# An attention and two MLPs on one core: the second head pair's loads of batch 0 are issued ahead of the first two pieces of MLP weights

## The chip, the cores and the metric

The kernel runs on one core of a Trainium2 chip. The metric is the device time of the whole program in microseconds (us); the kernel before takes 1157.22 us as the median of three runs (1156.96 to 1162.31).

## The reference

The inputs are q, k and v of shape (4 batches, 8 heads, 576 tokens, 64), all fp32.

```
out_up    = repeat(attention(mean-pooled q, k, v over 4 tokens), 4)   # 144 tokens
out_local = attention(q, k, v) with |row - col| < 4
x   = (out_up + out_local) as 2304 tokens x 512
h   = relu(x @ w_in)                 # w_in 512 x 2048
x   = (s * h * h + b) @ w_out        # first MLP, w_out 2048 x 512
out = ((x @ w_a) * (x @ w_b)) @ w2   # second MLP, d_ff 1536
```

Both attentions scale by 1/8 and use a softmax with its row maximum taken off and 1e-9 added to the sum.

## The kernel before

**Stages.** Heads are taken in pairs, so a batch has four pairs. The kernel first computes the attention of batch 0 alone (four pairs, overlapped with one another), and beside it brings in the weights of the first MLP and splits them. Then it runs the first MLP of batch m beside the attention of batch m+1, for all four batches, and last the second MLP. Each matrix product of the MLPs is three fp32r matmuls of high and low parts (hi·hi, hi·lo, lo·hi), and this is why weights have to be split: `hi` is the weight rounded to fp32r, `lo` the remainder.

**The first stage as steps.** The attention of one pair is laid out over steps `at` = 0 to 16, and pair p starts at step 11·p. At steps 0 to 3 TensorE turns q and k of the pair (L383, four transposes a step, read from `nat`), and ScalarE copies the result to `qT` and `kT` (L586). VectorE sums groups of four tokens (`pooledT`, L743). There are six score blocks j = 0 to 5 (two pooled, L407, and four local, L415), starting at steps 4, 6, 8, 9, 10 and 11. For block j, VectorE adds the mask (L755, local blocks), takes the maximum (L757) and the shift (L759); a step later ScalarE takes the exponentials (L598); another step later VectorE inverts the sums (L768, L770); GpSimd multiplies by them (L923); TensorE turns the result (L432, L436), ScalarE copies it (L607), TensorE multiplies with v (L446, L454), and VectorE takes the output (L777, L788). GpSimd also sums v over groups (L914, L917) at step 1 of a pair. Every engine runs its list of steps strictly in the written order.

**The weight pieces.** The first MLP's weights come in 16 pieces of 128 x 1024 fp32 (512 KB), through two buffers in `scratch` that alternate. A piece c is taken in two moves. At step 3(c+1), ScalarE (L622) and GpSimd (L928) each copy half of it to `hi`, after what they have to do for the attention in that step; both first wait for the piece's DMA. At step 3(c+1)+1 VectorE writes `lo` (L807), also at the end of its step, after waiting for both halves of `hi`. So piece 0 is wanted at step 3 by ScalarE and GpSimd and at step 4 by VectorE, pieces 1 and 2 at steps 6 and 9, and piece 3 at step 12.

**SP's queue.** All DMAs are issued by SP, in one written order. `load_pair(i, p)` issues 12 DMAs: four for q and k (L256), after waiting until the previous pair's four turns are done, two for v in groups (L259), and six for v in windows (L269). `load_piece(c)` issues one DMA (L279 for w_in, L284 for w_out); from c = 2 on it first waits until piece c-2 is wholly split (L273 to L275), because both share a buffer. The order of batch 0 before is: identity, pair 0, mask and two scalars (L294 to L296), pieces 0 and 1, pair 1, pieces 2 to 5, pair 2, pieces 6 to 9, pair 3, pieces 10 to 13, pieces 14 and 15, then pair 0 of batch 1. VectorE waits for the mask and both scalars before its first step. The first MLP begins on TensorE only when all 16 pieces are split and batch 0's attention is done.

The lines that hold the casts in place are, on ScalarE:

```
                if at % 3 == 0 and 0 < at // 3 <= NPIECE:
                    split_w_hi(at // 3 - 1)
```

on GpSimd the same, and on VectorE:

```
                if at % 3 == 1 and 0 < at // 3 <= NPIECE:
                    split_w_lo(at // 3 - 1)
```

Of the kernel before, what the change touches and what calls it, by code (L numbers as in the profile page):

```python
# [62 lines left out]
def build(nc, q, k, v, w_in, w_out, s, b, w_a, w_b, w2, mask_in, identity, out, o_dram):  # L63
# [6 lines left out]
    with stack:  # L70
# [177 lines left out]
        def _(sp):  # L248
            def load_pair(i, p):
                n = PAIRS * i + p  # L250
                past(sp, turn_ready, TURNS * n)
                for t, a in enumerate((q, k)):
                    for half in range(2):
                        dst = nat[:, t, half].rearrange("g r (h d) -> g r h d", h=2)
                        src = a.rearrange("b h (f g r) d -> b f g r h d", f=2, r=POOL)
                        sp.dma_start(dst, src[i, half, :, :, 2 * p:2 * p + 2, :]).then_inc(nat_in, 16)  # L256
                past(sp, vd_ready, n)
                for half in range(2):
                    sp.dma_start(vnat[:, half], groups_src(v, i, half, p)).then_inc(vnat_in, 16)  # L259
                if alone(i) and p == 0:  # L260
                    sp.wait_ge(vwin_clear, 1)
                past(sp, o_ready, NG * (n - 1))
                for w in range(NW):
                    lo_row = HALO if w == 0 else 0
                    hi_row = WK - HALO if w == NW - 1 else WK
                    t0 = WQ * w - HALO
                    src = v[i, 2 * p:2 * p + 2, t0 + lo_row:t0 + hi_row, :].rearrange("h t d -> t h d")
                    dst = vwin[lo_row:hi_row, p % 2, w, :].rearrange("t (h d) -> t h d", h=2)
                    sp.dma_start(dst, src).then_inc(vwin_in[p % 2], 16)  # L269

            def load_piece(c):
                if c >= 2:
                    sp.wait_ge(w_hi, c - 1)  # L273
                    sp.wait_ge(w_hi_pool, c - 1)
                    sp.wait_ge(w_lo, c - 1)  # L275
                if c < W1F // PIECE:
                    kd, part = divmod(c, FF1 // PIECE)
                    src = w_in[kd * P:(kd + 1) * P, part * PIECE:(part + 1) * PIECE]
                    sp.dma_start(piece_sb[:, c % 2, :], src).then_inc(piece_in[c % 2], 16)  # L279
                else:  # L280
                    f = (c - W1F // PIECE) * (PIECE // DM)
                    src = w_out[f * P:(f + PIECE // DM) * P, :].rearrange("(f p) m -> p f m", p=P)
                    dst = piece_sb[:, c % 2, :].rearrange("p (f m) -> p f m", m=DM)
                    sp.dma_start(dst, src).then_inc(piece_in[c % 2], 16)  # L284
# [9 lines left out]
            sp.dma_start(mask[:], mask_in).then_inc(consts_in, 16)  # L294
            sp.dma_start(s_col[:], s.partition_broadcast(P)).then_inc(consts_in, 16)
            sp.dma_start(b_col[:], b.partition_broadcast(P)).then_inc(consts_in, 16)  # L296
            load_piece(0)
            load_piece(1)
            for p in range(1, PAIRS):
                load_pair(0, p)  # L300
                for c in range(4 * p - 2, 4 * p + 2):
                    load_piece(c)
            load_piece(NPIECE - 2)
            load_piece(NPIECE - 1)
# [677 lines left out]
```

## Time and profile before

| | |
|---|---|
| median of three runs | 1157.22 us (1156.96 to 1162.31) |
| span of the profiled execution | 1150.5 us |
| own time of the profiled execution | not listed beside its span; the median of the runs is 6.7 us above the span |
| mean granted TensorE clock | 0.998 |
| TensorE matmuls busy | 1094.9 us (95%) |
| VectorE, ScalarE, GpSimd busy | 461.8, 422.7, 113.8 us |
| DMA | 52.43 MB, 91086 packets |
| the batch-0 stage | from 0 to about 111 us of the span |

All times of rows are microseconds from the start of the span. A line of the timeline gives start, duration, engine, source line, operation, and the output and input tensors, with the idle time of the engine just before it and what ended that idle time. SPq is SP's issuing of DMAs, so its duration is the issue and not the transfer. In the chain of waits each piece is the work, or the transfer in flight, that released the next one.

### The profile page before, as it was taken

Reading aid. Unit: us, or ns where it says so; the run is one execution under the profiler, and the core shown is the slowest. Engines: PE = TensorE matmul, PEld = TensorE weight load, DVE = VectorE, ACT = ScalarE, POOL = GpSimd, SP = SyncE. Lnnn points to the kernel's source line nnn. Section 1 sums busy time; section 2 is a strip of 40 time slices with the busy share of each in tenths; the row PEclk is TensorE's granted clock in tenths of the full one; section 3 lists DMA queues with packets and bytes.
Section 4 is the critical chain, followed back from the end, with each engine's and each line's share of the span. In section 5 each row is a group of like instructions: output and inputs, shape, how many; then the busy total and the mean of one; then the engine's idle time right before and its main releaser. Section 6 shows DMA issues by size and latency. Waiting matters only on the chain.

```text
span 1150.5 us, 19365 instructions
## 1 busy us (share of the span) xinstructions
PE 1094.9 (95%) x7048; PEld 1003.4 (87%) x7048; DVE 461.8 (40%) x1078; ACT 422.7 (37%) x1191; POOL 113.8 (10%) x149
## 2 busy tenths in 40 slices
PE   3887999999999999999999999999999999999998
PEld 3676899998989988999899998999989899999997
DVE  3766644455555455545533344421121211211211
ACT  3654544454445445445433343321121221211211
POOL 2433111210121112011100000000000000000000
PEclk9999999999999999999999999999999999999999
DMA  6443110112012101110040016201010010010000
GB/s 167 119 130 98 43 43 20 45 44 63 8 36 64 43 24 42 44 47 18 2 131 1 22 30 184 83 19 38 1 55 0 0 55 0 22 33 0 27 0 27
DMA packets 91086, 52.43 MB, mean 46 GB/s; under 512 B 59808, under 2 KB 84000, under 8 KB 91008
## 3 DMA queue, kind: packets, MB, share of 16 engines
q1 hardware_dynamic: 91008, 51.42, 16.1%
q8 instruction: 46, 0.75, 0.3%
q14 instruction: 32, 0.26, 0.1%
HBM read 41.97 MB, written 9.44 MB: 45 GB/s over the span
## 4 chain that ended last, share of the span: by engine, by line
PE 89%; SPq 3%; ACT 3%; DVE 3%; issue 1%; DMA 1%; DVEq 0%; ACTq 0%
PE bank L543 25%; PE bank L480 19%; PE bank L492 18%; PE bank L553 12%; PE bank L454 4%; PE bank L415 3%; PE bank L436 2%; PE bank L446 2%; PE bank L407 2%; PE bank L383 2%; SPq L256 1%; SPq L269 1%; PE bank L432 1%; ACT sm L598 1%; DVE lo L807 1%
## 5 line engine op out<-in xcount | busy, mean ns | idle before, releaser
L543 PE MATMUL bank<-x_hi,hi 128*128 128x384 f32 x576 | 193.9, 337 | 8.1 <-DVE prod L894 4.1
L543 PE MATMUL bank<-x_hi,lo 128*128 128x384 f32 x576 | 193.7, 336 | 0.0
L543 PE MATMUL bank<-x_lo,hi 128*128 128x384 f32 x576 | 193.4, 336 | 0.0
L480 PE MATMUL bank<-hi 128*128 128x288 f32 x512 | 160.7, 314 | 1.0 <-ACT scratch L649 1.0
L894 DVE TENSOR_TENSOR prod<-bank,a_sb 128x384 f32<-128x384 f32 x72 | 40.2, 558 | 293.4 <-ACT a_sb L711 293.4
L492 PE MATMUL bank<-g_hi,hi 128*128 128x288 f32 x512 | 157.8, 308 | 0.0
L480 PE MATMUL bank<-lo,hi 128*128 128x288 f32 x512 | 152.1, 297 | 0.0
L492 PE MATMUL bank<-g_lo,hi 128*128 128x288 f32 x512 | 151.8, 296 | 0.0
L480 PE MATMUL bank<-hi,lo 128*128 128x288 f32 x512 | 151.8, 296 | 0.0
L492 PE MATMUL bank<-g_hi,lo 128*128 128x288 f32 x512 | 150.9, 295 | 0.0
L830 DVE SCALAR_TENSOR_TENSOR scratch<-scratch,s_col 128x288 f32<-128x288 f32 x128 | 66.4, 519 | 189.4 <-ACT scratch L649 189.4
L711 ACT ACTIVATE a_sb<-bank 128x384 f32<-128x384 f32 x72 | 35.4, 492 | 290.8 <-PE bank L543 290.8
L649 ACT ACTIVATE scratch<-bank 128x288 f32<-128x288 f32 x128 | 52.7, 411 | 184.1 <-PE bank L480 184.0
L543 PEld LDWEIGHTS bank<-x_hi,hi 128*128 128x128 f32 x576 | 108.2, 188 | 13.7 <-ACT x_hi L644 6.0
L543 PEld LDWEIGHTS bank<-x_lo,hi 128*128 128x128 f32 x576 | 108.2, 188 | 3.1
L543 PEld LDWEIGHTS bank<-x_hi,lo 128*128 128x128 f32 x576 | 108.2, 188 | 0.0
L923 POOL TENSOR_TENSOR sm<-sm,den 96x306 f32<-96x306 f32 (+1 forms) x96 | 65.6, 684 | 423.7 <-DVE den L770 423.7
L480 PEld LDWEIGHTS bank<-hi 128*128 128x128 f32 x512 | 97.3, 190 | 6.1 <-issue 4.6
L492 PEld LDWEIGHTS bank<-g_hi,hi 128*128 128x128 f32 x512 | 96.6, 189 | 5.3 <-issue 4.8
L480 PEld LDWEIGHTS bank<-lo,hi 128*128 128x128 f32 x512 | 97.5, 190 | 0.0
L480 PEld LDWEIGHTS bank<-hi,lo 128*128 128x128 f32 x512 | 97.1, 190 | 0.0
L492 PEld LDWEIGHTS bank<-g_lo,hi 128*128 128x128 f32 x512 | 96.7, 189 | 0.0
(64 smaller groups left out, 1719.2 us busy)
## 6 DMA issues: line engine op xcount, KB each, us to landing
nat<-in_q SPq DMA_DIRECT2D x32, 144.0 KB
nat<-in_k SPq DMA_DIRECT2D x32, 144.0 KB
vnat<-in_v SPq DMA_DIRECT2D x32, 144.0 KB
o_transposed<-scratch SPq DMA_DIRECT2D x8, 576.0 KB, 3.5
o_raw<-o_transposed SPq DMA_DIRECT2D x6, 768.0 KB, 4.7
out<-y SPq DMA_DIRECT2D x18, 256.0 KB, 2.0
scratch<-in_moe_w_in SPq DMA_DIRECT2D x8, 512.0 KB, 4.4
scratch<-in_moe_w_out SPq DMA_DIRECT2D x8, 512.0 KB, 3.5
```

The lines of the kernel that those rows point to most:

```text
L383: mm = nc.tensor.transpose(turn_bank(i, t)[:, r * GH:(r + 1) * GH], nat[:, t // 2, t % 2, r, :], ident[0:GH, 0:GH])
L415: mm = nc.tensor.matmul(s_bank(i, j)[0:WQ, u * WK:(u + 1) * WK], qT[rows, w * WQ:(w + 1) * WQ], kT[rows, w * WQ:w * WQ + WK], start=True, ...
L454: mm = nc.tensor.matmul(o_bank(i, j)[e * D:(e + 1) * D, u * WQ:(u + 1) * WQ], vwin[:, p % 2, GW * half + u, e * D:(e + 1) * D], pts[:, j % ...
L480: mm = nc.tensor.matmul(HB[:, 0:HALF], wi(w, kd, f % F1), xs(x, h)[:, kd], start=(kd == 0 and n == 0), stop=(kd == KD - 1 and n == 2))
L492: mm = nc.tensor.matmul(ACC[o][:, 0:HALF], wo(w, f % F1, o), g[:, f % GB, :], start=(f % F1 == 0 and n == 0), stop=(f % F1 == F1 - 1 and n ...
L543: mm = nc.tensor.matmul(dst[:, 0:CH2], block2(w, f, j * KD + kd), x[:, kd, :], start=(kd == 0 and n == 0), stop=(kd == KD - 1 and n == 2))
L553: mm = nc.tensor.matmul(ACC[tt], x[:, f % GB, tt * P:(tt + 1) * P], rows2(w, f), start=(f == 0 and n == 0), stop=(f == F2 - 1 and n == 2))
L649: nc.scalar.activation(relu[:, f % 2, :], HB[:, 0:HALF], ACT.Relu).then_inc(r_ready, 1)
L711: nc.scalar.activation(a_sb[:, f % 2, :], HB[:, 0:CH2], ACT.Copy).then_inc(a_ready, 1)
L830: nc.vector.scalar_tensor_tensor(sq[:, f % 2, :], relu[:, f % 2, :], s_col[:, 0:1], relu[:, f % 2, :], ALU.mult, ALU.mult).then_inc(q_read ...
L894: nc.vector.tensor_tensor(prod[:, f % 2, :], SB[:, 0:CH2], a_sb[:, f % 2, :], ALU.mult)\
L923: nc.gpsimd.tensor_tensor(sm_view(j), sm_view(j), spread(den, j), ALU.mult).then_inc(p_ready, 1)
```

## The change

SP issues the twelve DMAs of batch 0's pair 1 before those of pieces 0 and 1. Nothing else moves: pieces 2 to 5 still follow, then pair 2, and no other engine's list changes.

```diff
             sp.dma_start(b_col[:], b.partition_broadcast(P)).then_inc(consts_in, 16)
-            load_piece(0)
-            load_piece(1)
             for p in range(1, PAIRS):
                 load_pair(0, p)
-                for c in range(4 * p - 2, 4 * p + 2):
+                for c in range(4 * p - 2 if p > 1 else 0, 4 * p + 2):
                     load_piece(c)
             load_piece(NPIECE - 2)
             load_piece(NPIECE - 1)
```

## Rows read from the trace of the kernel before

**Rows 1.** The page: busy time, share and instructions of each engine.
```profile
PE 1094.9 (95%) x7048; PEld 1003.4 (87%) x7048; DVE 461.8 (40%) x1078; ACT 422.7 (37%) x1191; POOL 113.8 (10%) x149
```

**Rows 2.** Chain of waits, 0 to 45 us: start, duration, what.
```profile
11.10 0.43 SPq L279
...
14.82 3.12 SPq L256
...
23.24 4.11 DMA scratch<-in_moe_w_in
27.34 0.02 issue
27.37 0.63 ACT hi L622
28.00 1.09 ACT sm L598 x6
...
30.66 0.69 PE bank L383 x4
...
32.37 0.91 ACT sm L598 x5
```

**Rows 3.** Timeline of SP's issues, from 0 to 50 us.
```profile
1.18 1.84 SPq L256 DMA_DIRECT2D nat<-in_q  x2
...
9.74 0.38 SPq L294 DMA_DIRECT2D mask<-band_mask  x1
...
38.39 1.68 SPq L256 DMA_DIRECT2D nat<-in_q  x2
...
47.09 2.26 SPq L279 DMA_DIRECT2D scratch<-in_moe_w_in  x2
```

**Rows 4.** Timeline of TensorE, the last turns of pair 0 and first pooled scores.
```profile
9.66 1.26 PE L383 MATMUL bank<-ident,nat 72*128 72x72 f32 x8 [0.29 <-ACT qT L586]
16.84 1.25 PE L407 MATMUL bank<-pooledT 64*72 64x144 f32 x8 [5.92 <-DVE pooledT L743]
```

**Rows 5.** The loads of w_in pieces (L279), issue to landing.
```profile
DMA to landing us min/median/max: 3.6/4.4/6.7
```

**Rows 6.** Timeline of ScalarE, 16 to 33 us.
```profile
16.64 0.63 ACT L622 ACTIVATE hi<-scratch 128x512 fp32r<-128x512 f32 x1 [4.99 <-DMA scratch<-in_moe_w_in]
18.97 0.38 ACT L598 ACTIVATE sm<-bank,shift 72x144 f32<-72x144 f32 x1 [1.71 <-DVE shift L759]
...
27.37 0.63 ACT L622 ACTIVATE hi<-scratch 128x512 fp32r<-128x512 f32 x1 [2.56 <-DMA scratch<-in_moe_w_in]
```

**Rows 7.** Timeline of VectorE, 18 to 32 us.
```profile
18.60 0.34 DVE L759 TENSOR_SCALAR shift<-mx 72x2 f32<-72x2 f32 x1
18.85 1.21 DVE L807 TENSOR_TENSOR lo<-scratch,hi 128x1024 fp32r<-128x1024 f32 x1
...
26.81 0.17 DVE L759 TENSOR_SCALAR shift<-mx 96x3 f32<-96x3 f32 x1
28.12 1.63 DVE L807 TENSOR_TENSOR lo<-scratch,hi 128x1024 fp32r<-128x1024 f32 x1 [1.14 <-POOL hi L928]
29.67 0.15 DVE L768 TENSOR_SCALAR den<-den 96x3 f32<-96x3 f32 x1
...
30.95 1.11 DVE L759 TENSOR_SCALAR shift<-mx 96x3 f32<-96x3 f32 x1
```

**Rows 8.** Timeline of GpSimd, 27 to 31 us.
```profile
27.97 0.69 POOL L923 TENSOR_TENSOR sm<-sm,den 96x306 f32<-96x306 f32 x1
...
30.76 1.27 POOL L914 TENSOR_TENSOR vnat<-vnat 72x512 f32<-72x512 f32 x1
```

**Rows 9.** Chain of waits, 97 to 119 us: the end of the stage.
```profile
109.26 1.24 DVE lo L807
110.50 0.50 issue
110.99 0.71 PE bank L383 x4
```

## The prediction

> **What bounds the kernel now.** I read the page first: TensorE's matmuls are busy for 95% of the span [rows 1], so a saving or a loss must reach TensorE's own order of work. The part that the diff touches lies in the first 111 us, where it does: TensorE's first MLP cannot start before the last piece of weights is split, and the chain ends this stage on VectorE's last `lo`, at 109.26, which releases TensorE at 110.99 [rows 9]. Whatever delays that point delays the end by as much, because behind it TensorE is nearly always busy and nothing there waits on a clock of its own.
>
> Then I read the chain of waits of the stage from its start. Up to 23.24 it runs through SP's issues one behind the other; then it is the flight of piece 2, 4.11 us; then ScalarE's cast of it at 27.37, exponentials, pair 1's turns at 30.66, exponentials at 32.37 [rows 2]. After that it is compute, with one more walk through SP. So at first sight SP's order matters and the nearest wait is for piece 2, not for pair 1.
>
> The engines' timelines give the slack. ScalarE waits 4.99 us for piece 0, casts it at 16.64, and waits 2.56 us for piece 2 [rows 6]. VectorE is not late for piece 0: it starts the first `lo` at 18.85, right behind its own shift, 1.58 us after the cast ended (16.64 + 0.63 = 17.27). For piece 2 it waits 1.14 us [rows 7].
>
> **The change part by part.** *Nothing is removed or added*: the same DMAs, casts and waits. Pair 1's twelve issues move 0.96 us earlier and two piece loads move later, past twelve issues.
>
> *Pair 1's loads earlier* buys nothing. They are first used at pair 1's turns at 30.66, and those follow ScalarE and TensorE work in the chain, not a DMA [rows 2]; I count 0, and since no row shows a wait for pair 1's data a gain is excluded. Their own first wait, the turns of pair 0, is over at 9.66 + 1.26 = 10.92, before the 11.10 at which SP gets there [rows 2, 4], so it costs 0 too.
>
> *When piece 0 is issued.* SP is free at 11.10. A pair's load took 9.74 - 1.18 = 8.56 us for pair 0 and 47.09 - 38.39 = 8.70 for pair 2 [rows 3], but from 12.05 (two piece issues behind 11.10) to 23.24, 11.19 us, for pair 1, with a single issue of 3.12 us in it, where its neighbours take about 0.9 [rows 2, 3]. That issue stood behind the 1 MB of two pieces just asked for; afterwards these are not ahead of it. I take the mean of pairs 0 and 2, 8.65 us: piece 0 is issued at 19.75 instead of 11.10. Bounds: 8.56 and 11.19, so 19.66 to 22.29.
>
> *When it lands.* Piece 2 is the same case, a piece straight behind a pair's twelve loads: 4.11 us [rows 2]. Piece 0 today takes 16.64 - 11.10 = 5.54 us, and the piece loads lie between 3.6 and 6.7 [rows 2, 5, 6]. I take 4.11, since the queue ahead of it will be that of piece 2: landing at 23.86. Bounds 3.6 and 5.54.
>
> The DMA page of the Trainium skill (DMA: Bandwidth & Descriptors, section "Anatomy of one DMA") fits a transfer as 2.0 us plus bytes over 436 GB/s, which for 512 KB is an estimate of 3.2 us. By it piece 0 would land 0.9 us sooner, and the sum below would be 0.9 us less. The row is above it, and no w_in piece of this trace was below 3.6; the sum goes by the row.
>
> *Who is held by it.* ScalarE runs in its written order, so at step 3 it stands in the cast of piece 0 until 23.86, and the exponentials of block 0 (18.97 today) are queued behind it. GpSimd stands in its own half. VectorE has its shift ready at 18.94 but stands in `lo` of piece 0, behind which are queued the sums of block 0 and the maxima of block 1. TensorE waits for block 0's exponentials. The cast takes 0.63, so it ends at 24.49, and VectorE follows 0.11 later, as it follows today's cast of piece 2 (28.00 to 28.12): 24.60 against 18.85. That is a delay of **5.75 us** at VectorE's first `lo` [rows 6, 7]. ScalarE's is 24.49 against 18.97, 5.5 us, so VectorE leads.
>
> *What absorbs part of it.* From 18.85 to the shift that starts at 26.81, VectorE is occupied nearly throughout and feeds ScalarE and TensorE, so all of it moves by 5.75. Next stands `lo` of piece 2. Today VectorE waits 1.14 us for that piece. Afterwards piece 2 can be issued once piece 0 is split: 24.60 + 1.21 = 25.81, about 25.9, landing at 30.0 by 4.11. ScalarE gets to it at 27.37 - 2.56 + 5.75 = 30.56, so the cast doesn't wait, and ends at 31.2. VectorE comes at 26.81 + 0.17 - 0.09 + 5.75 = 32.64 (its instructions start about 0.09 before the listed end of the one ahead [rows 7]), so its wait of 1.14 us is gone. It starts `lo` of piece 2 at 32.64 against 28.12: 4.52 us late.
>
> *A small gain.* That `lo` takes 1.63 us today and lies on GpSimd's multiplication at 27.97 to 28.66; the first one took 1.21 [rows 7, 8]. Afterwards the multiplication depends on sums that are ready at about 30.9 and is over by 31.6, so I take 1.21 - 1.63 = -0.42 (bounds -0.42 and 0). Delay behind it: 4.52 - 0.42 = **4.1 us**.
>
> Here a rule bears: SBUF — State Buffer of the Trainium skill, section "Who interferes with whom", says that a VectorE instruction with two SBUF inputs and a GpSimd one that reads SBUF exclude each other for the whole instruction. The 1.63 against 1.21 agrees. Without the rule, taking the 1.63 as it is, the sum would be 4.5 us.
>
> *Who carries the 4.1 on.* The chain before went through ScalarE's cast (which moves by only 31.2 - 28.0 = 3.2 us) to pair 1's first turn. The exponentials of block 5 at about 32.1 come behind both ScalarE's own order and the shift of 30.95 + 1.11 = 32.06 [rows 2, 7]. That shift moves by 4.1, so VectorE's path is the one that is last and the end moves by 4.1. Its 1.11 us, overlapped by GpSimd's sum at 30.76 [rows 8], stays as it is: both follow the same sums. Everything later (pairs 2 and 3, their waits on turns, the pieces' waits on splits) hangs on this point, and no later event in the stage has an origin outside it. I count 0 for later slack; bounds: 0, and 1.5 us given back.
>
> **Sum**: 8.65 (later issue) - 1.43 (landing 4.11 for 5.54) - 1.58 (slack of VectorE at piece 0) + 0.11 (following the cast) - 1.14 (wait for piece 2 gone) - 0.08 (start before listed end: 28.12 - 26.98 is 1.14, 28.12 - 26.89 is 1.23) - 0.42 = 4.1 us. Against the profiled span: 1150.5 + 4.1 = 1154.6. The runs' median is 6.7 us above that span, and nothing of it lies in the changed stage, so 1157.22 + 4.1 = **1161.3 us**, 0.35% slower. I treat 0.5% (5.8 us) as about what a measurement can tell from no change; so this is likely a real loss, but inside that bound.
>
> **Rivals.**
>
> *A. The long issue stays.* If the 3.12 us is not owed to the two pieces but to what else is in the queue (the mask and scalars are just ahead in both orders), pair 1 still takes 11.19 us, 2.5 more than in the sum: 4.1 + 2.5 = 6.6, 1163.8. With a landing of 5.54 it is 8.1, 1165.3. For it: that issue is in this very pair. Against: pair 0 and pair 2 have twelve issues without it.
>
> *B. The wait is hidden.* If pair 0's work could run on around piece 0, or later slack took it all, 1157.2. For it: the stage has idle time on every engine. Against: the cast is ahead of the exponentials in ScalarE's order, and each engine's order is fixed. Partial absorption, down to +2, belongs here. That the order of transfers doesn't change in effect (both sets are in flight together) would also end here, but 8.65 us of issue lie between.
>
> *C. Faster: SP's own stream is what counts.* The chain to 23.24 is SP's, and its 3.12 us issue is in it. If this shrinks to 0.9, SP arrives at piece 2 some 2.5 us sooner, the waits of 2.56 and 1.14 us for it vanish, and VectorE gains 1.14 + 0.42 = 1.6 us: 1155.6. It decides if piece 0 can land by 18.1, where VectorE's slack ends, and it is even at a landing of 19.8. The issue itself is not before 19.66, so only a transfer overtaking SP's issues, or ScalarE not standing in the cast, would bring it.
>
> **How the numbers follow.** Forecast (2.5 to 5.8 us later) 0.68; A (above 5.8) 0.20; B (from +2.5 down to 0) 0.10; C 0.02. The range: the lower end is issue and landing at their lower bounds (-0.1 - 0.5) with 1.5 us given back, 4.1 - 2.1 = +2.0, or 1159.2, widened to 1158.7 for the scatter of 0.3 and more between the runs; the upper end is A with a part of the longer landing, +7.6, or 1164.8. Chances: faster by over 0.5% 0.01 (C's 1.6 us would not reach it), within 0.5% 0.78 (forecast, B, most of C), slower by over 0.5% 0.21 (A and a little of the forecast's tail).
>
> **What would show it.** After: pair 1's issues from 11.10 in about 8.7 us without an issue of 3 us; piece 0 issued near 19.8; ScalarE's first cast near 23.9 with about 12 us idle ahead of it, ended by the DMA; VectorE's first `lo` near 24.6; no wait for piece 2 on ScalarE or VectorE; that `lo` near 32.6 and 1.2 us long; TensorE's first MLP matmuls about 4 us later than 111; the rest unchanged. A first cast before 20 would prove me wrong, and so would one past 26 or a start of the MLP moved by under 2 us.

## The result and the profile after

The changed kernel takes 1160.65 us (median of 20 runs, 1155.99 to 1165.59) against 1156.33 us of the kernel before (20 runs). The ratio is 1.0038 with a 95% interval of 1.0021 to 1.0054: 4.3 us slower, clear of noise, and less than 0.5%. Forecast were 4.1 us. The interval reaches from 2.4 to 6.2 us, so the run times confirm the sign and the rough size; the terms of the sum are checked in the profiles.

The numbers of the pages hardly differ from [rows 1]; line numbers behind the changed lines are two lower after. The page of the kernel after, busy time by engine:

```profile
PE 1096.5 (95%) x7048; PEld 1005.0 (87%) x7048; DVE 463.5 (40%) x1078; ACT 422.5 (37%) x1191; POOL 114.6 (10%) x149
```

The chain of waits of the kernel after, 0 to 45 us, answers to [rows 2]:

```profile
11.11 0.84 SPq L256
...
13.67 0.80 SPq L256
...
17.33 1.19 SPq L269
...
19.01 4.10 DMA scratch<-in_moe_w_in
23.11 0.05 issue
23.16 0.62 POOL hi L926
...
23.88 1.23 DVE lo L805
25.10 0.51 DVE den L766
```

The reader should see that the flight on the chain is now that of piece 0, at 19.01, where before it was that of piece 2, at 23.24, and that pair 1's fourth q/k issue takes 0.80 us where it took 3.12. Behind the flight come GpSimd's cast and VectorE's `lo` on the chain.

ScalarE's and VectorE's timelines of the kernel after, answering to [rows 6, 7]:

```profile
23.13 0.63 ACT L620 ACTIVATE hi<-scratch 128x512 fp32r<-128x512 f32 x1 [11.34 <-DMA scratch<-in_moe_w_in]
23.67 0.36 ACT L596 ACTIVATE sm<-bank,shift 72x144 f32<-72x144 f32 x1
...
30.17 0.61 ACT L620 ACTIVATE hi<-scratch 128x512 fp32r<-128x512 f32 x1
```
```profile
16.90 0.17 DVE L757 TENSOR_SCALAR shift<-mx 72x2 f32<-72x2 f32 x1
23.88 1.23 DVE L805 TENSOR_TENSOR lo<-scratch,hi 128x1024 fp32r<-128x1024 f32 x1 [6.81 <-POOL hi L926]
25.02 0.58 DVE L766 TENSOR_SCALAR den<-den 72x2 f32<-72x2 f32 x1
...
32.34 1.22 DVE L805 TENSOR_TENSOR lo<-scratch,hi 128x1024 fp32r<-128x1024 f32 x1
...
34.77 1.11 DVE L757 TENSOR_SCALAR shift<-mx 96x3 f32<-96x3 f32 x1
```

ScalarE idles 11.34 us for piece 0, and VectorE has its shift ready at 17.07 and stands for 6.81 us. ScalarE and VectorE don't wait for piece 2 any more: neither the cast at 30.17 nor the third `lo` at 32.34 has idle time ahead of it. (GpSimd idles 0.33 us for it, and its cast is over by 29.65, well ahead of that `lo`.) The end of the stage, from the chain of the kernel after, answering to [rows 9]:

```profile
112.51 1.24 DVE lo L805
113.75 0.45 issue
114.20 0.71 PE bank L381 x4
```

TensorE starts 3.2 us later than in the profile of before. The spans differ by more, 1156.1 against 1150.5. Most of the rest is the clock: over 60-us stretches the granted TensorE clock reads 1.00 except for single stretches at 0.97, of which the kernel before has one and this one has two. A stretch of 0.97 holds a short dip to the lower of the clock's two levels, 1.2 GHz instead of 2.4: in the kernel before the 4 us from 276 to 280 alone read 0.57. Of the kernel before, one such stretch and its neighbour (columns: the stretch and its length, busy time and instructions of each engine, granted clock, DMA share, GB/s):

```profile
240.00:300.00 60.00, 57.57 (x431) 52.38 (x430) 33.88 (x95) 30.89 (x108) 9.55 (x14) 0.97 0.15 38
300.00:360.00 60.00, 60.00 (x464) 54.91 (x463) 29.24 (x76) 27.18 (x83) 9.56 (x12) 1.00 0.15 37
```

and of the kernel after:

```profile
120.00:180.00 60.00, 58.01 (x433) 52.83 (x432) 31.18 (x87) 28.40 (x95) 8.38 (x11) 0.97 0.17 41
...
660.00:720.00 60.00, 55.44 (x350) 53.71 (x349) 25.53 (x33) 22.48 (x34) 0.00 (x0) 0.97 0.31 91
```

A stretch at 0.97 is 3% of 60 us, so one more of them costs an estimated 1.8 us of the 2.4 us that are left. Comparing runs of one mean clock takes this away. At 0.998 the five runs of the kernel after have a mean of 1157.4 us, and the kernel before, in 17 runs timed later with the experiments, 1153.2: a difference of 4.2 us, though not between runs timed together.

### The profile page after: what moved, and what is told of

It reads as the page before. It is cut to its first block, busy times and chain, and to the rows that moved or that the text cites. A ratio compares the mean times of both kernels' runs of the same rounds, so it can differ in the third digit from the quotient of the medians.

```text
span 1156.1 us, 19365 instructions
## 1 busy us (share of the span) xinstructions
PE 1096.5 (95%) x7048; PEld 1005.0 (87%) x7048; DVE 463.5 (40%) x1078; ACT 422.5 (37%) x1191; POOL 114.6 (10%) x149
## 4 chain that ended last, share of the span: by engine, by line
PE 89%; DVE 3%; ACT 3%; SPq 2%; DMA 2%; issue 1%; DVEq 0%; ACTq 0%; POOL 0%
PE bank L541 25%; PE bank L478 18%; PE bank L490 18%; PE bank L551 12%; PE bank L452 4%; PE bank L413 4%; PE bank L434 2%; PE bank L444 2%; PE bank L381 2%; PE bank L405 2%; SPq L256 1%; PE bank L430 1%; DVE lo L805 1%; SPq L269 1%; ACT sm L596 1%
```

## The experiments

All numbers of this table are starts on the timeline: of VectorE's `lo` of pieces 0, 3, 9 and 10, and of TensorE's first work behind the last split.

| kernel | piece 0 | piece 3 | piece 9 | piece 10 | TensorE | ratio (95%) |
|---|---|---|---|---|---|---|
| before | 18.85 | 35.93 | 70.82 | 77.53 | 110.99 | 1 |
| after | 23.88 | 39.75 | 74.65 | 80.79 | 114.20 | 1.0038 (1.0021 to 1.0054) |
| after, again | 24.23 | 40.10 | 75.01 | 82.94 | 116.36 | 1.0047 (1.0029 to 1.0064) |
| after, mask wait moved | 23.94 | 39.82 | 74.29 | 81.09 | 114.51 | 1.0040 (1.0024 to 1.0055) |
| one piece behind | 17.87 | 41.38 | 76.29 | 82.17 | 115.63 | 1.0048 (1.0028 to 1.0068) |
| casts later | 23.55 | 38.43 | 73.32 | 80.38 | 113.80 | 1.0032 (1.0012 to 1.0051) |
| only q, k ahead | 20.20 | 36.08 | 70.98 | 77.57 | 110.99 | 1.0008 (0.9985 to 1.0031) |
| before, mask wait moved | 16.92 | 34.77 | 69.75 | 77.38 | 110.80 | 0.9998 (0.9976 to 1.0020) |
| piece 2 early | 18.18 | 33.63 | 68.53 | 75.89 | 109.30 | 0.9944 (0.9924 to 0.9965) |
| both | 17.11 | 32.99 | 67.89 | 75.06 | 108.47 | 0.9960 (0.9943 to 0.9977) |
| both, and piece 10 | 16.64 | 33.31 | 68.22 | 74.41 | 107.28 | 0.9973 (0.9954 to 0.9993) |

From piece 3 to piece 9 all kernels take 34.9 to 35.0 us, but for the fourth row (34.5); from piece 10 to TensorE's start, 33.4 us, but for the last (32.9). So a kernel's loss or gain is fixed at piece 3, and the only place where it changes by much is between pieces 9 and 10 (5.9 to 7.9 us). Two of the kernels ("after, mask wait moved" and "both, and piece 10") were timed on another chip than the other experiments. Each ratio is to runs of the kernel before that were timed together with the kernel.

**The changed kernel again.**

> The changed kernel itself once more, to see how far its stages repeat. Theory: piece 0 lands at 23.1 to 23.9, TensorE's start behind the last split at 114.2 within 0.5 us, and the ratio to the kernel before 1.003 to 1.005. Rival (the 3.2 us at the end of the stage is chance of one profile): a start anywhere from 111 to 115.

It landed piece 0 at 23.48 and was 4.17 us behind at piece 3, against 3.82: that repeats. The start of TensorE doesn't: 116.36, not 114.20, outside the theory's half microsecond and above the rival's range too. Its chain shows why, 66 to 83 us:

```profile
76.89 5.28 DMA scratch<-in_moe_w_out
```

and the same flight, of piece 10 behind pair 3's loads, in the first profile of the kernel after:

```profile
76.40 3.61 DMA scratch<-in_moe_w_out
```

The end of the stage carries a scatter of some 2 us from this one flight. The reading to trust is that of piece 3.

**One piece behind.** Half of the change, as a diff against the kernel before.

```diff
             load_piece(0)
-            load_piece(1)
             for p in range(1, PAIRS):
                 load_pair(0, p)
-                for c in range(4 * p - 2, 4 * p + 2):
+                for c in range(4 * p - 2 if p > 1 else 1, 4 * p + 2):
```

> Piece 0 stays ahead of pair 1's loads, only piece 1 goes behind them. The number to look at is the start of TensorE's first work behind the last split (110.99 us before, 114.20 after). Theory (ScalarE, GpSimd and VectorE stand in their written order before a late piece): piece 0 lands near 16.6 as before, piece 1 is issued near 20.2 and lands near 24.3, VectorE's second lo starts near 25.0 instead of 21.0, and after the 1.1 us of wait for piece 2 and 0.4 us of overlap are given back, the start is 2.4 us later than before, near 113.4. Rival (only the first piece's lateness counts, later ones find slack): 111.0.

The mechanism holds and the size doesn't: the start is 4.6 us later, not 2.4, and at piece 3 the loss is 5.45 us, more than that of the whole change. SP's and ScalarE's timelines of this kernel:

```profile
13.15 3.54 SPq L256 DMA_DIRECT2D nat<-in_k  x2
...
21.76 21.24 SPq L279 DMA_DIRECT2D scratch<-in_moe_w_in  x5
```
```profile
17.12 0.63 ACT L621 ACTIVATE hi<-scratch 128x512 fp32r<-128x512 f32 x1 [5.41 <-DMA scratch<-in_moe_w_in]
27.14 0.63 ACT L621 ACTIVATE hi<-scratch 128x512 fp32r<-128x512 f32 x1 [8.44 <-DMA scratch<-in_moe_w_in]
```

With one piece ahead, three quarters of the long issue are back (the two k issues take 3.54 us, against 4.17 with two pieces ahead and 1.63 with none), so piece 1 is issued at 21.76 and not at 20.2, and its flight is 5.4 us and not 4.1. Both were mis-sized in the expectation. The 8.44 us of idle time stand at the second cast, so a late second piece is paid for as well, and the rival (only the first piece's lateness counts) falls.

**Only q and k ahead.** `load_pair` is cut in two functions, `load_qk` and `load_v`. The order, against the kernel before:

```diff
+            load_qk(0, 1)
             load_piece(0)
             load_piece(1)
-            for p in range(1, PAIRS):
+            load_v(0, 1)
+            for c in range(2, 6):
+                load_piece(c)
+            for p in range(2, PAIRS):
```

> Only the four q and k loads of pair 1 go ahead of pieces 0 and 1; its eight v loads stay behind them. Theory (VectorE has 1.6 us of slack at piece 0, and SP is then free for piece 2 some 2.5 us sooner because no 3 us issue comes up): piece 0 is issued near 14.5 and lands near 18.6, the first lo starts near 19.35, 0.5 us late, the wait of 1.14 us for piece 2 goes, and TensorE's start moves to 109.9, 1.1 us sooner than before. Rival (any lateness of piece 0 is paid in full): 0.5 to 2 us later, 111.5 to 113.

Neither: 0.15 us late at piece 3, and 110.99 at the end, as before. Piece 0 was issued at 14.26 as expected, but flew 5.2 us and landed at 19.45, so the first `lo` was 1.35 us late. The second was 1.78 late, the third 0.55 and the fourth 0.15, so the wait for piece 2 took it up. Slack of this size is there, and the rival, that any lateness is paid in full, falls. The theory's gain of 1.1 us failed because SP did not come to piece 2 sooner (22.85, against 23.24 in the kernel before): the k issues were short, but the six issues of v windows behind the two pieces took 6.44 us where they took 3.86. The hold-up had moved to them:

```profile
16.27 6.44 SPq L271 DMA_DIRECT2D vwin<-in_v  x6
```

**Casts later.** The order of loads of the changed kernel, with the casts elsewhere in the lists; the diff is against that kernel.

```diff
+                if at in (6, 8):
+                    split_w_hi((at - 6) // 2)
-                if at % 3 == 0 and 0 < at // 3 <= NPIECE:
+                if at % 3 == 0 and 2 < at // 3 <= NPIECE:
                     split_w_hi(at // 3 - 1)
```

(on ScalarE and GpSimd; VectorE's `lo` at 7 and 9 in the same way)

> The order of loads of the changed kernel; but the casts of pieces 0 and 1 stand at steps 6 and 8 and their lo at 7 and 9 of every engine's list, instead of 3, 6 and 4, 7. Theory (the cost is the place of the cast in a fixed order, in front of block 0): exponentials of block 0 run near 17.2 instead of 23.7, piece 0 still lands near 23.1, VectorE has block 1's maxima done before it, and TensorE's start is 1.5 us sooner than in the changed kernel, near 112.7. Rival (transfers of pair 1 and the pieces get in each other's way, whatever the casts' place): 114.2.

Piece 0 arrived about as late as in the changed kernel, and ScalarE had block 0's exponentials done before it, at 16.95:

```profile
22.80 0.63 ACT L620 ACTIVATE hi<-scratch 128x512 fp32r<-128x512 f32 x1 [5.03 <-DMA scratch<-in_moe_w_in]
```

The loss at piece 3 shrank from 3.82 to 2.50 us. The cast was 0.33 us earlier than in the changed kernel, so 1.0 to 1.3 us of the loss was the place of the cast in a fixed order, with the same DMAs in the same order. The other 2.5 us remain because the piece is still late at its new place: ScalarE idles 5.03 us and VectorE 4.82 us for it, and ScalarE another 0.82 us for piece 2. No run moved the casts further back. The start at 113.80 is only 0.4 us sooner than the 114.20, since the interval from piece 9 to 10 was 7.06 us here and 6.14 there.

**Mask wait moved**, in the kernel before and in the changed one.

```diff
                 if j >= POOLED:
+                    if alone(i) and p == 0 and j == POOLED:
+                        dve.wait_ge(consts_in, 48)
...
-            dve.wait_ge(consts_in, 48)
```

> The kernel before, but VectorE waits for the mask and the two scalars at its first masked block instead of at its start. Theory (SP's walk to piece 2 sets the time of the kernel before, not VectorE): the first pooled sums start near 11.7 instead of 15.4, the first lo near 17.4 instead of 18.85, and ScalarE just waits longer for piece 2, so that TensorE's start behind the last split stays at 111.0 within 0.3 us. Rival (VectorE's own chain sets it): 1.5 us sooner, 109.5.

> The changed kernel, with VectorE waiting for the mask and scalars only at its first masked block. Theory (in the changed kernel VectorE stands at its first lo for the cast of piece 0, with 6.8 us idle): the pooled sums start near 11.8 instead of 13.7, the idle time grows by as much, and the first lo (23.9) and the fourth (39.8) stay within 0.4 us. Rival (VectorE's early start counts there too): up to 1.9 us sooner at both.

In the changed kernel the first `lo` stood 9.66 us for the cast and stayed at 23.94, the fourth at 39.82: VectorE's early start buys nothing there. In the kernel before, the first `lo` came 1.9 us sooner and the third 1.2, with ScalarE still waiting 2.87 us for piece 2. These 1.2 us are not the edit's, as far as the profile shows: SP's issues ahead went quicker in this profile and reached piece 2 at 22.30 and not 23.24. The start moved by only 0.2 us, since the interval from piece 9 to 10 was 7.63 us here and 6.71 in the kernel before, and the ratio is 1.

**Piece 2 early.** If SP's walk to piece 2 bounds the kernel before, then the right thing to move is piece 2.

```diff
             load_piece(0)
             load_piece(1)
-            for p in range(1, PAIRS):
+            load_qk(0, 1)
+            load_piece(2)
+            load_v(0, 1)
+            for c in range(3, 6):
+                load_piece(c)
+            for p in range(2, PAIRS):
```

> The kernel before, but piece 2 is issued between the q,k loads and the v loads of pair 1. Theory: SP waits for the first lo until 20.1, piece 2 lands near 24.4 at the latest instead of 27.4, the waits of 2.6 and 1.1 us for it go, and TensorE's start moves from 111.0 to 109.5 (1.14 us of wait and 0.42 us of overlap). Rival (piece 2 is hidden anyway, or the later v loads are missed): 111.0 or later.

> The two edits together: VectorE's wait for the mask moved back, and piece 2 issued ahead of pair 1's v loads. Theory (each hides the other's gain): first lo near 17.4, piece 2 issued near 18.7 and landed near 22.9, TensorE's start near 108.0, 3.0 us sooner than before, and the whole 0.25% faster. Rival (no more than the second edit alone): 109.5.

Piece 2 was issued at 19.50; ScalarE's third cast and the third `lo` have no idle time ahead, and piece 3 is 2.30 us sooner, the start 1.7. Of the 2.30, 0.67 were there at the first `lo` already, from quicker issues, which leaves 1.6 for the edit. VectorE's timeline of this kernel, with the wait of [rows 7] gone:

```profile
26.22 1.23 DVE L818 TENSOR_TENSOR lo<-scratch,hi 128x1024 fp32r<-128x1024 f32 x1
```

With both edits it is 2.94 us at piece 3 and 2.5 at the start. The intervals of the two ratios overlap, and their middles stand the other way round, so that "both" beats the one edit rests on one profile of each. The times gained more than the starts did: 0.56% is 6.5 us (interval 4.0 to 8.8, six runs) beside 1.7 us at the start, and 0.40% is 4.6 us (2.7 to 6.6) beside 2.5. A part may be that the one profile of the kernel before caught a short flight of piece 10 (3.5 us, against up to 5.4 in others) and so an early start; the rest is not explained.

**And piece 10.** The same order in pairs 2 and 3, as a diff against the kernel with both edits.

```diff
             for p in range(2, PAIRS):
-                load_pair(0, p)
-                for c in range(4 * p - 2, 4 * p + 2):
+                load_qk(0, p)
+                load_piece(4 * p - 2)
+                load_v(0, p)
+                for c in range(4 * p - 1, 4 * p + 2):
```

> The two edits of the sixth kernel, and in pairs 2 and 3 too the next piece (6 and 10) is issued between the q,k loads and the v loads. Theory (the stage has one more place where SP's walk through a pair's loads is last: piece 10 behind pair 3, flights of 3.5, 3.6 and 5.3 us in three profiles, and an interval of 6.1 to 7.9 us between the tenth and eleventh lo): the tenth lo stays near 67.9, the interval shrinks to 5.9 as behind pair 2, TensorE's start is near 107.2 instead of 108.5, and it no longer scatters. Rival (ScalarE and TensorE are last there as well): 108.5.

The start came at 107.28, 3.7 us before that of the kernel before, as expected. At the mean clock of 0.998, four runs average 1149.5 us and four of the kernel before, timed together with them, 1152.5. It is faster than the kernel before and than the changed one; against "both" the ratios (0.9973 and 0.9960) don't tell the two apart. Its piece 9 to 10 took 6.19 us, and no engine waited for piece 10, whose `lo` took 1.21 us and not 1.63; one profile can't say that the scatter is gone. At piece 2 the order did not do what it does in the two kernels ahead: that load, asked for at 17.98, was in flight for 6.76 us, and ScalarE idled 1.70 us for it, so that piece 3 came 0.3 us later than in "both". Its chain of waits:

```profile
17.98 6.76 DMA scratch<-in_moe_w_in
```

So asking for a piece ahead of the v loads takes the wait away in two profiles of three.

## Why the prediction was right, step by step

- *Pair 1's loads earlier, 0*: right. No profile puts an engine's wait down to them.
- *Later issue, +8.65*: measured 19.01 - 11.10 = 7.91, which is 0.74 less and below the lower bound of 8.56. The long q/k issue is gone, as forecast, but the term was read from pairs 0 and 2, whose six v-window issues took 3.87 and 4.00 us; here they took 3.38. (Their mean is also 8.63, not 8.65.) Over all profiles pair 1's two k issues took 3.5 to 4.7 us where one or two pieces stood just ahead of its q and k (six profiles), and 1.63 where none did (five). Rival A, as a long issue without the pieces ahead, fell. Its thought that something else in the queue plays a part stays open: at pairs 2 and 3 a piece stands just ahead as well, and there the two k issues took 1.6 to 2.4 us, and once 3.2.
- *Flight, 4.11*: measured 4.12 here and 4.6 in the second profile. That it can be 5.4 with one piece ahead, or 5.2 behind q and k alone, was within the bounds (3.6 to 5.54) but not foreseen, and the 6.76 us of piece 2 in the last kernel lie beyond them. The fit that the prediction quotes from the Trainium skill (DMA: Bandwidth & Descriptors, section "Anatomy of one DMA") is given there for DMAs issued by GpSimd, and these are SP's. The estimate of 3.2 us from it is below the flight of every piece straight behind a pair's loads that ScalarE waited for (3.5 to 5.4 us in ten profiles), so going by the row was right.
- *VectorE's slack and the following of the cast, -1.58 + 0.11*: the landing moved by 6.49 us and the first `lo` by 5.03, so -1.46: right.
- *Not in the sum*: the pieces now land close together, and GpSimd's cast of piece 1 lies on VectorE's sum (0.58 us for 0.15 before, the row at 25.02). That is +0.43 at the second `lo`, which the prediction put at nothing.
- *Wait for piece 2 gone, -1.14 and -0.08*: the delay fell from 5.46 to 4.22, so -1.24. Right.
- *The shorter third `lo`, -0.42*: 1.22 for 1.63, and the delay fell to 3.82 at piece 3. The trace agrees with the rule of the Trainium skill (SBUF — State Buffer, section "Who interferes with whom"): GpSimd's multiplication (30.75 to 31.44) was over before this `lo`.
- *The sum*: 7.91 - 1.42 - 1.46 + 0.43 - 1.24 - 0.40 = 3.82, against 4.1. That it comes so near is in part luck: the issue term was 0.74 us too large and the 0.43 us left out offset more than half of it.
- *Nothing later*: right from piece 3 to 9 (34.90 us against 34.89). Between pieces 9 and 10, 0.6 us were given back in the first profile and 1.2 us lost in the second, by chance of a flight. The prediction saw one more walk through SP behind 45 us, but counted nothing for it, on the ground that no later event has an origin outside this point; the flight of piece 10 is such an event. Its sum fits the point that repeats, and the end only within that scatter.
- *Rival B* (hidden) is excluded by the 3.8 us at piece 3 and by the interval. *Rival C* pointed at the right resource and the wrong move: SP's walk did bound the kernel before, and taking piece 2 through it sooner gained 1.6 us at piece 3 (the changed kernel lost 3.8 there).
- *What lies around the span, 6.7 us*: that was a profiled run at a high mean clock beside a median at a lower one. The profiled run of the kernel after took 1157.86 for a span of 1156.1, so 1.8 us lie around it, and the rest of the 6.7 is between runs. The forecast of 1161.3 stands on the 1157.22 of three runs; over 20 runs the kernel before has 1156.33.

## What to carry to other kernels

A load that no one is waiting for is not improved by being asked for sooner, and it is paid for by whatever it is put ahead of: look for the waits that end at each load in the queue, and order by these. Where engines run a fixed list, a late operand stops everything behind its first use, so its price is its lateness minus the slack there, less what later waits take up. In a stage of joins, compare kernels at the last point that repeats, not at the end.

## What was not expected of the hardware

- The issue of a q/k load takes 0.80 us, but pair 1's fourth took 2.70 us behind one piece and 3.12 behind two (the kernel before). SP's issuing can be held up by what it has asked for, and with the pieces behind q and k the hold-up came at the v windows (6.44 us for 3.86).
- A piece issued straight behind a pair's loads, where ScalarE waited for it, flew between 3.5 and 5.4 us; piece 2 behind q and k alone flew 6.8 us in one profile. What sets it was not found: it was not the number of pieces asked for together (piece 0 flew 6.2 us with no piece behind it, and 5.5 with piece 1 behind it).
- A later request can hold up an earlier one. VectorE's first sums start when the second scalar lands. From its issue that is 4.7 and 4.6 us with two pieces asked for behind it (the kernel before and "piece 2 early"), 4.0 us with one, and 3.4 to 3.5 us in the four kernels with q and k behind it.
- The granted clock reads 1.00 in this first stage and right behind it, but TensorE's first twelve L480 matmuls take 2.97 us, and the same twelve a few us later 1.66. The first ones start every 0.24 us with 288 columns each, which is 1.2 columns per ns, the rate of the lower level (1.2 GHz); the later ones start every 0.13 us, 2.2 per ns, near the upper level (2.4 GHz). So the column doesn't show everything. The chain of the kernel before, 97 to 119 us:

```profile
111.70 2.97 PE bank L480 x12
...
116.49 1.66 PE bank L480 x12
```

- The times of the kernel before follow their mean granted clock, by about 0.9 us for each 0.001 (a line through 77 runs, 0.990 to 0.998).
